# Retention: swapped partition halves for every second head, and first-layer tiles run whole

## The reference, cut

```python
# q, k, v: (2, 8, 576, 64)
scores = (1 / sqrt(64)) * q @ k.T
gamma  = 1 - 2 ** (-5 - arange(8))
ret    = scores * where(rel >= 0, gamma ** rel, 0)      # rel = query position - key position
x      = (ret @ v)  as (1152, 512)
p      = domain_probs / (domain_probs.sum(-1) + 1e-9)
x      = sum over e of p[:, e] * (relu(x @ w1[e]) @ w2[e])        # w1: (4, 512, 1024)
h      = x @ w_in                                                  # (512, 2048)
out    = (h * tanh(softplus(h))) @ w_out
```

## Time and profile before

| | us |
|---|---|
| three runs, median (lowest to highest) | 632.7 (630.49 to 634.12) |
| the profiled execution | 630.54 |
| its span, first to last instruction | 628.8 |
| PE busy in the span | 620.6 |
| GpSimd busy in the span | 284.4 |

### The profile page before, as it was taken

How to read it: one execution, slowest core, us unless ns; L and a number is a source line. 1 busy time by engine, 2 the same in 40 slices (tenths; PEclk the granted TensorE clock), 3 DMA queues, 4 the chain that set the end, 5 groups by cost and what they waited for, 6 DMA issues and landing times.

```text
span 628.8 us, 9476 instructions
## 1 busy us (share of the span) xinstructions
PE 620.6 (99%) x3764; PEld 553.7 (88%) x3765; DVE 243.5 (39%) x388; ACT 238.0 (38%) x459; POOL 284.4 (45%) x239
## 2 busy tenths in 40 slices
PE   8999999999999999999999999999999999999997
PEld 5788899998999999899999899989979999999996
DVE  5756743333143333143323143335564333314324
ACT  3555433332223432223432223435544455334432
POOL 4759535543435542535543535532553544443300
PEclk9999999999999999999999999999999999999999
DMA  8954312222112322102321202321100232201002
GB/s 275 339 177 158 111 34 68 100 88 64 51 35 67 101 84 67 51 34 67 101 84 56 62 35 67 101 67 47 55 34 34 68 116 85 68 0 52 1 0 100
DMA packets 25146, 50.41 MB, mean 80 GB/s; under 512 B 2896, under 2 KB 3216, under 8 KB 25104
## 3 DMA queue, kind: packets, MB, share of 16 engines
q1 hardware_dynamic: 24816, 49.66, 24.2%
q10 hardware_dynamic: 288, 0.17, 0.1%
HBM read 47.45 MB, written 2.36 MB: 79 GB/s over the span
## 4 chain that ended last, share of the span: by engine, by line
PE 95%; DVE 3%; ACT 1%; issue 0%; POOL 0%; DVEq 0%; ACTq 0%; POOLq 0%
PE bank L480 30%; PE bank L482 30%; PE bank L481 30%; PE bank L434 2%; PE bank L474 2%; DVE xt L896 1%; PE bank L612 1%; PE bank L605 1%; PE bank L438 1%; DVE acc_sb L866 0%; DVE acc_sb L870 0%; ACT h_hi L708 0%; DVE h_lo L826 0%; DVE acc_sb L975 0%; ACT h_act L691 0%
## 5 line engine op out<-in xcount | busy, mean ns | idle before, releaser
L381 POOL TENSOR_TENSOR w_lo<-w_raw,w_hi 128x512 fp32r<-128x512 f32 x96 | 128.8, 1356 | 151.0 <-ACT w_hi L354 151.0
L482 PE MATMUL bank<-w_hi,h_lo 128*128 128x512 f32 x432 | 169.9, 393 | 0.0
L481 PE MATMUL bank<-w_lo,h_hi 128*128 128x512 f32 x432 | 169.5, 392 | 0.0
L480 PE MATMUL bank<-w_hi,h_hi 128*128 128x512 f32 x432 | 169.0, 391 | 0.0
L376 POOL TENSOR_TENSOR ws<-ws_f,ws 128x1024 fp32r<-128x1024 f32 x24 | 57.9, 2412 | 150.4 <-ACT ws L350 150.4
L853 DVE TENSOR_TENSOR h_act<-part,bank 128x384 f32<-128x384 f32 x96 | 52.8, 550 | 179.4 <-PE bank L482 179.4
L482 PEld LDWEIGHTS bank<-w_hi,h_lo 128*128 128x128 f32 x432 | 81.0, 188 | 17.5
L481 PEld LDWEIGHTS bank<-w_lo,h_hi 128*128 128x128 f32 x432 | 81.0, 188 | 9.8
L480 PEld LDWEIGHTS bank<-w_hi,h_hi 128*128 128x128 f32 x432 | 81.1, 188 | 9.6
L703 ACT ACTIVATE h_hi<-h_act 128x384 fp32r<-128x384 f32 x64 | 33.6, 526 | 104.8 <-DVE h_act L853 104.8
L713 ACT ACTIVATE part<-bank 128x384 f32<-128x384 f32 x72 | 35.2, 489 | 82.9 <-PE bank L482 82.2
(11 more groups left out here) (87 smaller groups left out, 916.0 us busy)
## 6 DMA issues: line engine op xcount, KB each, us to landing
w_raw<-in_weights SPq DMA_DIRECT2D x144, 256.0 KB, 2.7
qkv<-in_chunks SPq DMA_DIRECT2D x18, 512.0 KB, 4.9
out<-acc_sb SPq DMA_DIRECT2D x6, 256.0 KB, 2.0
out<-acc_sb SPq DMA_DIRECT2D x1, 768.0 KB, 5.3
consts<-in_consts ACTq DMA_DIRECT2D x1, 146.0 KB, 3.8
ident<-in_consts SPq DMA_DIRECT2D x1, 64.0 KB, 4.0
consts<-in_consts SPq DMA_DIRECT2D x1, 34.0 KB, 4.0
p_nat<-in_probs ACTq DMA_DIRECT2D x1, 18.0 KB, 3.9
```

The costliest lines, as they stand in the source:

```text
L381: pool.tensor_tensor(w_lo[:, layer, x], w_raw[:, r % RAW], w_hi[:, layer, x].bitcast(F32), ALU.subtract).then_inc(s_wl, 1)
L480: pe.matmul(out, w[0], x[0], start=first, stop=False, **more)
L481: pe.matmul(out, w[0], x[1], start=False, stop=False, **more)
L482: return pe.matmul(out, w[1], x[0], start=False, stop=last, **more)
```

## The change

Heads are taken in pairs. In a slot, the even head of a pair (x = 0) keeps tokens on partitions 0 to 63 and features on 64 to 127; the odd one (x = 1) has them the other way round (TOK, FEAT). Scores of a chunk then fill all 128 partitions of a bank, 256 columns wide; states lie in banks 4 (x = 0) and 5 (x = 1). What follows from the layout:

- `masked` becomes two operations of 64x256; `state_copy` stays at two, one for each x.
- `v_decay` of chunks 2 to 17 becomes one operation over all 128 partitions. It multiplies the key features, too, by ones in the table. For chunks 0 and 1 it is two operations on 64 partitions, each after the one before.
- since the decay rewrites the features which the scores read, the score block waits for the decay of chunk c+1 (`scaled(n)`), from chunk 2 on.
- the score block waits for both state copies at its start.
- the tables of half tiles go; tile t runs whole in turn 8 + t, between score block and output block. Turns 16 to 18 have none.
- the tables' part for the keys is loaded for 128 partitions.

The core of the diff:

```diff
+TOK = (slice(0, CH), slice(CH, P))
+FEAT = (slice(CH, P), slice(0, CH))
+ALONE = 2
+def scaled(c):
+    return 2 * (c + 1) if c < ALONE else ALONE + c + 1
-AFTER_SCORES = {8: (0, 1), 9: (1, 1), 10: (2, 1), 11: (3, 1), 12: (4, 1), 13: (5, 0), 14: (5, 1),
-                15: (6, 0), 16: (6, 1), 17: (7, 0), 18: (7, 1)}
-AFTER_OUTPUT = {7: (0, 0), 8: (1, 0), 9: (2, 0), 10: (3, 0), 11: (4, 0)}
-HIDDEN_IN = {t: c for c, (t, half) in AFTER_SCORES.items() if half}
+HIDDEN_IN = {8 + t: t for t in range(UNITS)}
...
-        ps_s = [banks[i][KEYS, :].rearrange("p (h c) -> p h c", h=HEADS) for i in range(SCORES)]
-        ps_state = [banks[i][FEATS, 0:HS * DH].rearrange("p (h c) -> p h c", h=HS) for i in range(2)]
+        ps_s = [banks[i][:, 0:PAIRS * CH].rearrange("p (h c) -> p h c", h=PAIRS) for i in range(SCORES)]
+        ps_state = [banks[4 + x][FEAT[x], 0:PAIRS * DH].rearrange("p (h c) -> p h c", h=PAIRS) for x in range(2)]
...
-            sp.dma_start(consts[KEYS, 0:ROW0], consts_in[KEYS, 0:ROW0]).then_inc(s_const, 16)
+            sp.dma_start(consts[:, 0:ROW0], consts_in[:, 0:ROW0]).then_inc(s_const, 16)
...
+            def scores_head(c, hp, x):
+                return pe.matmul(ps_s[c % SCORES][TOK[x], hp], by_feats(c, 0, x)[:, hp], by_feats(c, 1, x)[:, hp],
                                  start=True, stop=True)
+            def state_head(c, hp, x):
+                return pe.matmul(ps_state[x][:, hp], by_tokens(c, 1, x)[:, hp], by_tokens(c, 0, x)[:, hp],
+                                 start=(c % PER_BATCH == 0 and hp == 0), stop=True, skip_group_check=True)
             def scores_and_state(c):
                 n = c + 1
                 if n < CHUNKS:
                     pe.wait_ge(s_slot[n % SLOTS], landed(n))
+                    if n >= ALONE:
+                        pe.wait_ge(s_vd, scaled(n))
                     if n >= SCORES:
-                        pe.wait_ge(s_sm, n - SCORES + 1)
+                        pe.wait_ge(s_sm, 2 * (n - SCORES + 1))
                 if has_state(c):
-                    pe.wait_ge(s_vd, c + 1)
-                for h in range(HEADS):
-                    if has_state(c) and c > 0 and h % HS == 0:
-                        pe.wait_ge(s_st, 2 * states(c - 1) - 1 + h // HS)
+                    pe.wait_ge(s_vd, scaled(c))
+                    if c > 0:
+                        pe.wait_ge(s_st, 2 * states(c - 1))
+                for hp in range(PAIRS):
+                    for x in range(2):
...
             for c in range(TURNS):
                 if c < CHUNKS:
                     scores_and_state(c)
-                if c in AFTER_SCORES:
-                    plain_half(*AFTER_SCORES[c])
+                if c in HIDDEN_IN:
+                    s, i = divmod(HIDDEN_IN[c], ITEMS)
+                    plain_ready(s, i)
+                    plain_products(s, i)
                 if c == 0:
                     keep_warm(3)
                 if c > 0:
                     output(c - 1)
-                if c in AFTER_OUTPUT:
-                    plain_half(*AFTER_OUTPUT[c])
...
+                for x in range(2):
+                    act.activation(by_feats(c + 1, 0, x), ps_state[x], ACT.Copy).then_inc(s_st, 1)
...
-                dve.tensor_tensor(by_keys(c, 1), ps_s[c % SCORES], mask.unsqueeze(1).broadcast_to([CH, HEADS, CH]),
-                                  ALU.mult).then_inc(s_sm, 1)
+                for x in range(2):
+                    dve.tensor_tensor(by_tokens(c, 1, x), ps_s[c % SCORES][TOK[x]],
+                                      mask[TOK[x]].unsqueeze(1).broadcast_to([CH, PAIRS, CH]), ALU.mult)\
+                       .then_inc(s_sm, 1)
...
             def v_decay(c):
                 pool.wait_ge(s_slot[c % SLOTS], landed(c))
-                v = by_keys(c, 0)
-                pool.tensor_tensor(v, v, key_decay[KEYS, c % PER_BATCH].unsqueeze(2).broadcast_to([CH, HEADS, DH]),
-                                   ALU.mult).then_inc(s_vd, 1)
+                if c >= ALONE:
+                    both = qkv[:, c % SLOTS, 0]
+                    if c == ALONE:
+                        pool.wait_ge(s_vd, scaled(c - 1))
+                    pool.tensor_tensor(both, both, key_decay[:, c % PER_BATCH].unsqueeze(3)
+                                       .broadcast_to([P, 2, PAIRS, DH]), ALU.mult).then_inc(s_vd, 1)
...
+    for x in range(2):
+        of_keys = np.ones((CH, PER_BATCH, 2, PAIRS))
+        of_keys[:, :, x] = keys[:, :, x::2]
+        consts[TOK[x], 0:MASK0] = of_keys.reshape(CH, MASK0)
```

More of the change, by code:

```diff
@@ L275, in build, with by_tokens, by_feats @@
         s_out = sem("s_out")
[L277 to L281, removed]
+        def by_tokens(c, which, x):
+            return qkv[TOK[x], c % SLOTS, which, x]
+        def by_feats(c, which, x):
+            return qkv[FEAT[x], c % SLOTS, which, x]
         def landed(c):
@@ L498, in plain_ready, with plain_products @@
                     pe.wait_ge(s_cc, ITEMS * (sums(s) - 1) + (C21, C12)[i] + 1)
-            def plain_products(s, i, tiles):
+            def plain_products(s, i):
                 t = ITEMS * (s % STAGES) + i
-                for k in tiles:
+                for k in range(KT):
                     at = slice(P * k, P * (k + 1))
@@ L506, in plain_products @@
                                (xa_hi[:, k], xa_lo[:, k]), k == 0, k == KT - 1)
-                if KT - 1 in tiles:
-                    mm.then_inc(s_l1, 1)
-            def plain_half(t, half):
-                s, i = divmod(t, ITEMS)
-                if half == 0:
-                    plain_ready(s, i)
-                plain_products(s, i, range(2 * half, 2 * half + 2))
+                mm.then_inc(s_l1, 1)
             def product(s, j):
@@ L616, in _ @@
             pe.wait_ge(s_slot[0], landed(0))
-            for h in range(HEADS):
-                mm = scores_head(0, h)
+            for hp in range(PAIRS):
+                for x in range(2):
+                    mm = scores_head(0, hp, x)
             mm.then_inc(s_sc, 1)
@@ L655, in _ @@
                         plain_ready(s, i)
-                        plain_products(s, i, range(KT))
+                        plain_products(s, i)
                         if e == MOE_EXPERTS:
@@ L731, in _ @@
                     state_copy(c)
[L732 to L734 removed]
+                if c in HIDDEN_IN:
+                    plain_hi(*divmod(HIDDEN_IN[c], ITEMS))
                 if c > 0:
@@ L1015, in tables @@
     keys = gamma[None, None, :] ** (MID - CH * c[None, :, None] - i[:, None, None])
-    consts[KEYS, 0:MASK0] = keys.reshape(CH, MASK0)
-    consts[KEYS, MASK0:ROW0] = i[:, None] <= i[None, :]
+    for x in range(2):
+        of_keys = np.ones((CH, PER_BATCH, 2, PAIRS))
+        of_keys[:, :, x] = keys[:, :, x::2]
+        consts[TOK[x], 0:MASK0] = of_keys.reshape(CH, MASK0)
+        consts[TOK[x], MASK0:ROW0] = i[:, None] <= i[None, :]
     rows = gamma[:, None] ** (i[None, :] - MID) / np.sqrt(DH)
@@ L1031, in by_tokens, with chunks @@
     def by_tokens(a):
-        return a.reshape(BATCH, HEADS, PER_BATCH, CH, DH).transpose(0, 2, 3, 1, 4).reshape(CHUNKS, CH, HEADS, DH)
+        a = a.reshape(BATCH, PAIRS, 2, PER_BATCH, CH, DH).transpose(0, 3, 4, 2, 1, 5)
+        return a.reshape(CHUNKS, CH, 2, PAIRS, DH)
     def by_features(a):
-        return a.reshape(BATCH, HEADS, PER_BATCH, CH, DH).transpose(0, 2, 4, 1, 3).reshape(CHUNKS, DH, HEADS, CH)
+        a = a.reshape(BATCH, PAIRS, 2, PER_BATCH, CH, DH).transpose(0, 3, 5, 2, 1, 4)
+        return a.reshape(CHUNKS, DH, 2, PAIRS, CH)
+    def chunks():
+        tokens = np.stack([by_tokens(v), by_tokens(k)], axis=2)
+        feats = np.stack([by_features(k), by_features(q)], axis=2)
+        upper = np.stack([tokens[:, :, :, 0], feats[:, :, :, 1]], axis=3)
+        lower = np.stack([feats[:, :, :, 0], tokens[:, :, :, 1]], axis=3)
+        return np.concatenate([upper, lower], axis=1)
     def halves(w1, w2):
```

63 lines of the change are left out of this document (28 added, 35 removed).

## The result

| | before | changed |
|---|---|---|
| median (lowest to highest), us | 631.47 (630.49 to 634.12), 6 runs | 638.07 (636.26 to 638.83), 6 runs |
| profiled execution, us | 630.54 | 636.62 |
| its span, us | 628.8 | 634.6 |

The ratio is 1.0089, with a 95% interval of 1.0061 to 1.0117. The change makes the kernel slower by 0.9%; the prediction was 638.0 us in a range of 632.5 to 643.

The account below looks back on a forecast made before the run. PE bounds the kernel; in the opening stage the decay gate delays it. Summed turn starts put the second layer at 65.95 against 60.36 (+5.6, or +4.5 without the stall); +5.3 on the 632.7 median gives 638.0 us, range 632.5 to 643.

Parts of the forecast that it names:

- The gate: Score blocks wait for GpSimd's decay, queued behind weight remainders: 4.1 us from end of turn c-2 to start of turn c.
- The chain ahead of turns 7 and 8: Output block through VectorE, ScalarE, GpSimd's remainder and decay: 4.1 us, so turn 7 starts at 24.25, turn 8 at 27.3.
- Turns 2 to 6: Waiting for both state copies makes these turns 2.05 us instead of about 1.8; turn 6 starts at 20.15.
- off the path: VectorE's two masks, at most 2 x 0.43 instead of 0.68, add under 0.2 us a turn beside PE's work, except last turns.
- the price of the copies: Two state copies on ScalarE take 0.65 us, so the score block's wait ends about 0.3 later.
- The first turn: PE starts turn 1 at 9.9 instead of 9.49, waiting for chunk 2's decay behind the split decays.
- The saved entries of tiles: Eight whole tiles instead of halves save 0.20 us each, 1.6 on PE; a whole tile takes 2.30.
- The stall of turn 6: PE's unexplained 1.38 us stop inside turn 6's output block was kept, so turn 6 ends at 23.2.
- Turn 8: Starts at 27.3, 4.1 us after turn 6's end at 23.2; turn 9 follows 4.0 later at 31.3.
- The tail: After turn 16's start no tile covers VectorE: about 4.75 us until the second layer at about 65.95.
- Quarters and banks: Score block stays at 1.08 us: two quarters, not four; changes of quarter owner and bank sharing taken to cost nothing.

Follow-up runs that it names:

- the run with the gate alone: Kernel before, plus only the score block's wait for the decay of its chunk, from chunk 2 on; 637.55 us, ratio 1.0093.
- early decays: Changed kernel with each decay issued one turn earlier on GpSimd, ahead of a turn's weight remainders, still over 128 partitions; ratio 1.0013.

## Why the prediction was right, step by step

- **The gate.** The mechanism is as worked out, and the run with the gate alone shows that it is the cause. The decay takes 1.04 us on 128 partitions as on 64 (two of 16 took 1.26 and 1.23, both beside VectorE's work). In turns 9 to 13 it only just bites: starts 3.98 to 4.05 apart, (47.75 - 31.69)/4 = 4.02 on average, where 4.1 stood. PE's own work is 3.98, but 3.66 in turn 10 in both kernels without the gate (31.64 to 35.30 with decays of token quarters only, 32.45 to 36.11 with early decays), where the output of a batch's first chunk needs no state. So the gate costs 0.4 in turn 10, in which no row names a wait. Turn 14, behind two remainders, came 5.23 after turn 13, where 5.34 stood. The longest wait is the one before turn 7 (2.55), and not those before turns 8 and 14 (0.64 and 1.16) as forecast: turn 5 ended 0.6 us late and the chain behind it was dearer (next point), while turn 6, without the stall, ended when it was expected to.
- **The chain ahead of turns 7 and 8.** Here the step failed. I used the 4.1 us read behind turn 9, and it took 4.9: turn 5 ends at 21.16 - 0.45 = 20.71 and turn 7 starts at 25.62; turn 6 ends at 25.62 - 2.55 = 23.07 and turn 8 starts at 28.03, 4.96 later. Where no tile lies between, VectorE still has the masks ahead of the scaling. This is the scaling behind turn 5:

```profile
21.60 0.42 DVE L809 TENSOR_TENSOR x_tmp<-bank,row_decay 128x256 f32<-128x256 f32 x1
```

It starts 0.89 after PE's output block, where it is 0.19 in the earlier trace rows, and the decay of 24.30 took 1.23 in place of 1.04. These two, with a start of PE 0.09 behind the decay's end instead of 0.19, make the 4.9 ahead of turn 7. Ahead of turn 8 GpSimd itself is the limit: it runs from 23.07 to 27.93 without rest, at 1.23 and 1.44 for operations of 1.04 and 1.27.

- **Turns 2 to 6.** The direction was right, the term was too small: 2.21 a turn and turn 6 at 21.16, where 2.05 and 20.15 stood, +1.0. The 1.8 of today was read from turn 2 alone; turns 1 to 5 of the kernel before take (18.92 - 9.49)/5 = 1.89 on average, so the change added 0.33 a turn where 0.25 stood. The step that failed is "off the path" for the masks and the price of the copies: both pairs change partition half between their operations and lose 0.13 each, and VectorE's loop (0.91 masks, 0.91 to the split, 0.39 split) is as long as PE's.
- **The first turn.** 10.10 against 9.9.
- **The saved entries of tiles.** 2.28 for a whole tile, 2.30 expected; 0.22 saved for each instead of 0.20.
- **The stall of turn 6.** I kept 1.38 us and it was not there: turn 6 went from 21.16 to 23.06, 1.90 where 3.05 stood. This took back the error of turns 2 to 6, so that turn 6 ended at 23.07 against 23.2. That is luck: nothing in the prediction says why the stall should go.
- **Turn 8.** 28.03 against 27.3, and the next turn 3.66 later instead of 4.0, because of the short score block. So turn 9 came at 31.69 against 31.3, and the turns of 4.02 instead of 4.1 brought turn 13 to 47.75 against 47.7.
- **The tail.** 5.30 from turn 16 to the second layer, 4.75 expected (its terms add up to 4.67). The masks, 0.87 for two, and their place ahead of the last scalings are in it.
- **Quarters and banks.** A score block with a state stayed at 1.08 (36.75 - 35.67). The Trainium skill (TensorEngine Tiling (Array Packing), Gotcha 1: PSUM Pressure) says that different row tiles cannot use the same PSUM bank at once. No run here shows a cost of it: the block is 1.08 in both layouts, and that of turn 8, in which both row halves write one bank, is the one that shrank, to 0.61.

The sum holds errors of about 1 us each, of both signs, and they cancel down to 66.24 against 65.95. That 638.0 met 638.07 is luck beyond that. The forecast put 5.3 us on a base of 632.7, the median of three runs; with six runs the base is 631.47, so the medians differ by 6.6, and the profiled executions by 6.1. A base 1.2 too high covered a loss sized too small. The 5.3 was itself taken between 5.6 and 4.5, the latter for the case that the stall goes; it did go, and the stage still lost 5.9. The sign and the mechanism the runs confirm.

## What to carry to other kernels

When an operation comes to touch data that an engine reads earlier than before, ask what is queued ahead of it on its own engine, and follow that chain back to the waiting engine itself: a chain that begins with PE's own last block can't be outrun by PE. Move such an operation ahead of its queue in the same edit. Pairs of small operations that alternate between partition halves cost more than pairs on one half (0.13 us a pair here), and work that fills a gap must stay where the gap is.

## What the runs showed of the hardware

**The clock falls in some executions.** Mean granted clocks of one kernel's executions were 1.0, 0.997 and 0.995. For the kernel before, in the series beside the run with five whole tiles, the ten executions at 0.999 or 1.0 have a median of 631.6 us, the nine at 0.997 have 633.1, the four at 0.995 have 635.1. Much of the scatter of this kernel goes with that. The profiled execution of the run with the mask in two shows one case (us of stretch, busy us of PE, PEld, DVE, ACT, POOL with instructions, granted clock, DMA share, GB/s):

```profile
23.00:26.00 3.00, 1.51 (x23) 1.41 (x22) 3.00 (x5) 0.66 (x3) 2.86 (x3) 1.00 1.06 348
26.00:30.00 4.00, 4.00 (x25) 3.24 (x23) 1.37 (x4) 0.92 (x2) 2.26 (x2) 0.60 0.69 240
30.00:34.00 4.00, 4.00 (x41) 3.40 (x42) 1.55 (x4) 1.43 (x3) 1.24 (x2) 0.54 0.65 234
34.00:38.00 4.00, 4.00 (x62) 3.37 (x58) 2.06 (x5) 2.08 (x5) 1.02 (x2) 1.00 0.16 31
```

PE was busy for 1.51 of 3.0 us, and in the next 8 us it was granted 0.60 and 0.54, that is mostly 1.2 GHz in place of 2.4; a half tile took 2.28 from start to end instead of 1.32. The kernel with the gate alone had the same after its waits at turns 7 and 14. But a wait is not enough for it: in the changed kernel's profiled execution PE was busy for 0.45 of the 3.0 us from 23 to 26, and the clock stayed at 1.00. So a wait early in the kernel may cost more than itself, in some executions; what decides it no run here shows.

**A stall that names nothing.** In the kernel before, and in four of the runs, PE stops for 1.0 to 1.8 us inside the output block of turn 6, after two or three records (1.38 in the earlier trace rows). It was absent from the changed kernel and from seven others. No run was made to find its cause; it stays open.
